# Three fills of unread transposes taken out from between TensorE's first orders

## What is computed

```python
# 1: a causal convolution of 7 taps, whose weights differ by token and head (8 heads)
w = exp(weight_gen - max); w = w / (sum(w) + 1e-9)
x = sum over k of w[..., k] * x_pad[token + k]          # x_pad: 6 rows of zeros ahead

# 2: two mixes with the token before, a feed-forward layer (d_ff 1024), a gate
xk = mu_k * x + (1 - mu_k) * x_prev
xr = mu_r * x + (1 - mu_r) * x_prev
k = maximum(xk @ w_k, 0);  v = (k * k) @ w_v
y = sigmoid(xr @ w_r) * v

# 3: up to 1024, a convolution of 3 taps along the tokens, a gate, back to 192
h = maximum(y @ w_in, 0)
out = (h * sigmoid(conv3(h, conv_w))) @ w_out
```

## Time and profile before

| | |
|---|---|
| time, median of 3 runs | 717.82 us (717.74 to 718.28) |
| the profiled execution, its time | 718.39 us |
| its span in the trace | 716.6 us |
| TensorE busy | 706.2 us (99%) |
| VectorE busy | 668.5 us (93%) |
| ScalarE busy | 634.9 us (89%) |
| transposes of L964 | 88 in all, the first at 4.0 us, the last at 72.7 us |

### The profile page before, as it was taken

How to read it: one execution, slowest core, us unless ns; L and a number is a source line. 1 busy time by engine, 2 the same in 40 slices (tenths; PEclk the granted TensorE clock), 3 DMA queues, 4 the chain that set the end, 5 groups by cost and what they waited for, 6 DMA issues and landing times.

```text
span 716.6 us, 10616 instructions
## 1 busy us (share of the span) xinstructions
PE 706.2 (99%) x3537; PEld 601.3 (84%) x3537; DVE 668.5 (93%) x982; ACT 634.9 (89%) x1280; POOL 3.6 (0%) x12
## 2 busy tenths in 40 slices
PE   7999999999999999999999999999999999999998
PEld 7777788888888888888887888888888888888998
DVE  6999999999999999999999999999999999987686
ACT  4998998999989899897999989998998989898975
POOL 1000000000000000000000000000000000000000
PEclk9999999999999999999999999999999999999999
DMA  9502010200202020020200102020110202000001
GB/s 257 189 27 96 1 55 1 55 23 2 78 1 77 1 77 1 1 79 0 78 1 14 65 1 78 1 78 1 26 53 1 77 1 73 1 22 1 24 1 49
DMA packets 10107, 29.86 MB, mean 42 GB/s; under 512 B 1326, under 2 KB 4936, under 8 KB 9926
## 3 DMA queue, kind: packets, MB, share of 16 engines
q1 hardware_dynamic: 9244, 28.89, 12.4%
q10 hardware_dynamic: 810, 0.30, 0.2%
HBM read 21.75 MB, written 6.39 MB: 39 GB/s over the span
## 4 chain that ended last, share of the span: by engine, by line
PE 81%; DVE 14%; issue 3%; ACT 2%; POOL 0%; DVEq 0%; POOLq 0%; ACTq 0%
PE up L424 34%; PE od L537 19%; PE dn L509 4%; PE dn L493 4%; PE dn L516 4%; PE dn L513 4%; PE dn L512 4%; PE dn L515 3%; DVE att L2103 2%; DVE prod L2085 2%; DVE gat L2236 2%; DVE cv L2208 2%; PE od L964 2%; PE mid L348 2%; DVE cv L2221 1%
## 5 line engine op out<-in xcount | busy, mean ns | idle before, releaser
L537 PE MATMUL od<-wo_sb,gat 128*128 128x192 f32 x1024 | 181.7, 326 | 0.1
L537 PEld LDWEIGHTS od<-wo_sb,gat 128*128 128x128 f32 x1024 | 169.9, 190 | 6.4 <-ACT o_sb L1111 0.4
L2167 DVE TENSOR_TENSOR kq_lo<-ksq,kq_hi 128x512 fp32r<-128x512 f32 (+2 forms) x136 | 90.3, 666 | 15.1 <-ACT kq_hi L1053 14.1
L1082 ACT ACTIVATE cv<-h,prm 128x512 f32<-128x512 f32 x128 | 91.7, 716 | 10.9 <-DVE gat L2236 10.3
L2208 DVE SCALAR_TENSOR_TENSOR cv<-h,prm,cv 128x512 f32<-128x512 f32 x128 | 94.9, 749 | 3.5 <-ACT cv L1082 2.4
L2221 DVE SCALAR_TENSOR_TENSOR cv<-h,prm,cv 128x512 f32<-128x512 f32 x128 | 95.6, 749 | 0.6
L2236 DVE TENSOR_TENSOR gat<-h,cv 128x512 f32<-128x512 f32 (+1 forms) x136 | 89.0, 664 | 5.2 <-ACT cv L1100 3.4
L2085 DVE TENSOR_TENSOR prod<-xin,wgt 128x768 f32<-128x768 f32 (+1 forms) x100 | 93.3, 934 | 0.0
L2103 DVE TENSOR_TENSOR att<-att,prod 128x768 f32<-128x768 f32 (+1 forms) x97 | 91.2, 941 | 0.1
L1074 ACT ACTIVATE h<-up 128x512 f32<-128x512 f32 (+2 forms) x136 | 77.4, 570 | 13.9 <-PE up L424 13.8
L1100 ACT ACTIVATE cv<-cv 128x512 f32<-128x512 f32 (+1 forms) x136 | 81.6, 605 | 5.1 <-DVE cv L2221 4.4
(11 more groups left out here) (137 smaller groups left out, 1362.2 us busy)
## 6 DMA issues: line engine op xcount, KB each, us to landing
xin<-in_x SPq DMA_DIRECT2D x14, 960.0 KB, 4.8
out<-o_sb SPq DMA_DIRECT2D x16, 384.0 KB, 3.9
wgt<-in_weight_gen SPq DMA_DIRECT2D x1, 1092.0 KB, 14.2
h<-h SPq DMA_DIRECT2D x1, 1024.0 KB, 4.5
xin<-in_x SPq DMA_DIRECT2D x1, 864.0 KB, 4.4
h<-in_moe_w_v SPq DMA_DIRECT2D x1, 768.0 KB, 10.2
wo_sb<-in_moe_w_out SPq DMA_DIRECT2D x1, 768.0 KB, 15.7
h<-in_moe_w_k SPq DMA_DIRECT2D x1, 512.0 KB, 7.1
```

The costliest lines, as they stand in the source:

```text
L537: mm = nc.tensor.matmul(o, tile[:, b * P:(b + 1) * P], wo_sb[:, c, :], start=(c == 0 and b % 2 == 0), stop=(c == NC - 1), skip_group_check ...
L1082: nc.scalar.activation(conv_tile(w, c), win(w, c, 0), ACT.Copy, scale=prm[:, 3 + NC + c:4 + NC + c])\
L2167: nc.vector.tensor_tensor(ring(kq_lo, c, n), ring(ksq, c, n), ring(kq_hi, c, n).bitcast(F32), ALU.subtract).then_inc(kql_ok, 1)
```

## The change

Three calls of `warm` are deleted from the list of TensorE's first orders: those of 3, 11 and 16 transposes. The two at the very start, of 30 and 28, stay. No other step, no wait and no other engine's list is touched.

```diff
@@ -561,7 +561,6 @@
                 r_part(0, 1)
                 r_part(0, 2)
                 up1(0, 4)
-                warm(3)
                 down1(0, 0)
                 up1(0, 5)
                 down1(0, 1)
@@ -577,7 +576,6 @@
                 down1(0, 5)
                 down1(0, 6)
                 down1(0, 7)
-                warm(11)
                 up2(0, 0)
                 up2(0, 1)
                 up2(0, 2)
@@ -606,7 +604,6 @@
                 t_part(2, 2)
                 down1(1, 6)
                 down1(1, 7)
-                warm(16)
                 up2(1, 0)
                 up2(1, 1)
                 up2(1, 2)
```

## The result

| | before | changed |
|---|---|---|
| median | 717.92 us (20 runs) | 718.96 us (20 runs) |
| lowest to highest | 717.58 to 718.33 us | 717.70 to 719.85 us |
| runs with a mean granted clock of 1.0 | see below | 3 |
| runs with a mean granted clock of 0.998 | see below | 17 |

The ratio is 1.0014, with a 95% interval of 1.0008 to 1.0021. The median lies in the forecast range (717.2 to 721.2 us), and the move is smaller than the 0.2% that the prediction took as its bound. But it is a real loss of 1.04 us where none was forecast. The median is in the range only because the range was drawn out over Rival A; the sum behind the forecast put this effect at 0.

What follows compares the result with a forecast made beforehand. TensorE's own list was taken to bound the kernel. Direct savings of 0 + 0 + 0 us and 0 us for the clock left the median of before, 717.8 us, as forecast; range 717.2 to 721.2 us.

Steps and rivals of the forecast that it cites:

- Rival A: Behind the 16 at 72 us: the clock falls, 3.0 us slower, 720.8 us; chance 0.20.
- Direct effect: At all three fills: removing them saves 0 us, with 0.4 us as the most the rows leave room for.
- the three terms: Fills at 31, 42 and 72 us: 0 us saved at each, at most 0.10, 0.15 and 0.15 us.
- Rival C: At the fills: waits served sooner without them, 0.4 us faster, 717.4 us; counted within the 0.58 for no effect.
- this term: TensorE's clock over the emptied gaps at 42 and 72 us: stays up, 0 us lost.
- The rival's lower figure: Behind the 16 at 72 us: clock back in half the time, 719.3 us; no separate chance.
- Rival B: Behind both 42 and 72 us: the clock falls twice, 5.0 us slower, 722.8 us; chance 0.12.
- a fall after the 11 alone: Behind 42 us only: 2.0 us slower after 1.0 us of cover, 719.8 us; chance 0.06.

Runs made afterwards that it cites:

- no16: Kernel before with only the 16 transposes at 72 us taken out: 719.18 us median, ratio 1.0011.
- only11: Changed kernel with the 11 transposes at 42 us put back, the 3 and 16 still out: 719.28 us median, ratio 1.0013.
- half11: Kernel before with 5 transposes in place of the 11, and no 3 or 16: 719.68 us median, ratio 1.0013.
- behind42: Kernel before with the 11 replaced by 3 transposes in the waits behind the first matmuls at 42 us: 718.08 us median, ratio 1.0005.
- four72: Kernel before with 4 transposes in place of the 16 at 72 us: 717.89 us median, ratio 1.0001.
- no11: Kernel before with only the 11 transposes at 42 us taken out: 718.02 us median, ratio 1.0006.
- after2: The changed kernel run again, all three fills out, against the kernel before: 718.43 us median, ratio 1.0010.

## Why the prediction was wrong

**Direct effect, 0 us: right.** Each of the three terms holds, as far as the times can tell. The runs of the changed kernel without a fall take 717.70 to 718.03 us, within the spread of before. The matmul on y_lo starts as far behind VectorE as before, the waits of 0.25, 0.37 and 0.48 us are the same, and the idle times ahead of the first matmuls are 1.13 and 1.61 us where about 1.2 and 1.6 us were named. Rival C, the gain of up to 0.4 us, did not show.

**"I take 0 for this term, because the nearest row, at 25.91 us, lost nothing": this step failed.** The gap of 1.20 us at 25 us loses nothing in any of the 99 runs of before, but the gap of 1.13 us at 42 us costs the clock in 5 of 11 and that of 1.61 us at 72 us in 19 of 33 (`no16`, `only11`, `half11`). I had written that both are thinner behind and that no row shows so thin a stretch, and then let the nearest row decide the size of the term. It was nearest by the length of the gap, and that was not enough. What sets the gap at 25 us apart isn't shown: `behind42`, with more work behind the gap, still had 4 falls in 11, and `four72`, with 1.17 us idle at 72 us, had none. The sentence that this gap is no longer than some at full clock in this trace also holds for 42 us alone: behind its start the kernel before has one idle time of TensorE of this size, the 1.20 us at 25.91 us, and none like the 1.61 us at 72 us. One profile was also too little for it: `no11` has the same idle time to the hundredth as the changed kernel, and no fall in its profiled execution. Even a row of exactly this gap at full clock would not have shown that it is safe.

**The forecast was a choice between fall and no fall.** The prediction gave each outcome one chance, as if the kernel had only one. It has several: with both gaps open, 8 of 31 runs had no fall, 22 had one and 1 had two. The median of the first 20 moved by 1.04 us because 17 of them had one.

**Rival A had the mechanism, half of the place and twice the price.** It named the gap at 72 us; in the profiled execution the fall came behind 42 us, and the experiments show both. Its 3.0 us rested on 6 us at the lower level. That row is TensorE coming from rest at the start of the kernel, and it is not a constant either: in `no11` the fills are at full pace from about 7 us on, 3 us after the first. Between work, the lower level lasted 3.41 us in `no16` and from 43.9 to 47.2 us in the changed kernel, and cost 1.55 and 1.36 us. The rival's lower figure, for a clock back in half the time, was 1.5 us and fits the 1.55 us.

**Rival B had too much cover.** Its form with a fall after the 11 alone, with a chance of 0.06, is what the profiled execution shows. I estimated that 1.0 us of a fall behind 42 us would be hidden by ScalarE's table loads. They hid nothing: TensorE was 1.36 us late ahead of them and 1.39 us behind them. In the chain ScalarE's steps stand right behind TensorE's sixteen matmuls, and its table loads started 1.38 and 1.39 us later than before, so its part was pushed back whole. A stretch in which another engine bears the chain is cover only if what that engine does doesn't hang on the late one.

**Which rule of the Trainium skill held.** Its page "TensorE: Matmul & The Clock Gate", section "A second HAM failure mode: psum-queue depth-cycling", says that short idle times between groups of matmuls can make the clock go back and forth. The traces agree in part: idle times of 1.13 and 1.61 us were each followed by a fall in about half of the executions, but by one fall that did not repeat, where the page tells of idle times that recur. Section "Part 4: PE-mode transpose" of the same page says that the full clock doesn't engage for transposes. The runs disagree once more, since 5 transposes in one gap and 8 or 4 in the other took the falls from about half of the runs to none in 11 each.

## What to carry to other kernels

A fill that nobody reads can be free and still worth its place, because what it holds is the clock of the matmuls behind it. Look for gaps of TensorE of about 1 us or more with further waits right behind. Price a fall from rows at the lower level in the middle of the work (here 1.36 and 1.55 us), not from the start of the kernel, and grant no cover from engines that themselves wait for TensorE.

A gap at full clock in one profile proves nothing, since the same gap fell in about half of the executions. Count over many runs, by the mean granted clock, which here told 0.998 from 1.0 where a median of 11 (`no11`: 1.0006) told nothing. A quarter to a half of the fill (4 or 8 of 16, 5 of 11) had no fall in 11 or 22 runs, which doesn't exclude a rare one; and less of it wins nothing, so there is no reason to be sparing.

## What was not expected of the hardware

The clock's rise at the start, too, comes at another point in each execution. In the changed kernel the fills are still at the lower level (421 ns) up to 9.4 us. These are its fills between 7.2 and 9.5 us, durations min/median/max, then first and last start:

```profile
L961 PE MATMUL od<-ident x13: 404/421/421, 6.9 to 9.4; 128*128 128x128 f32 x13
```

and those of `no11` between 7.3 and 9.5 us, with the same work ahead of them:

```profile
L963 PE MATMUL od<-ident x20: 272/273/327, 7.1 to 9.5; 128*128 128x128 f32 x20
```

In `no11` the full clock is there more than 2 us earlier, and the first matmul behind the gap at 42 us starts at 42.09 instead of 42.63 us. So one and the same list of steps meets the clock's moments of change at different points.

The first 30 fills take the longer the later the clock rises, and that gives a measure for every profiled execution. These are their rows in two executions of the changed kernel, first the one with the fall at 42 us, then that of `after2`, which had none:

```profile
4.05 6.23 PE L961 MATMUL od<-ident 128*128 128x128 f32 x30 [4.05 <-POOL ident L329]
4.06 5.49 PE L961 MATMUL od<-ident 128*128 128x128 f32 x30 [4.06 <-POOL ident L329]
```

Seven profiled executions have at least one gap without any fill ahead of its first matmul. In the two with a fall, of the changed kernel and of `no16`, these fills took 6.23 and 6.22 us; in the five without one (`no11`, `only11`, `half11`, `behind42`, `after2`) they took 4.83 to 5.49 us. In the kernel before they took 6.40 us without a fall, so a late rise does nothing where the gaps are filled. That fits a gap that falls only when it meets the clock at a bad moment. But seven executions are few, and no experiment moved the gaps against the clock's rise, so this link is argued and not shown.
